# Attention, its fallback and the experts in one block instead of three, with the last tiles' work in another order

## The reference, cut to what matters

```python
def _attn_ref(q, k, v, f_logit):                 # (4, 8, 768, 48) each
    f = 1.0 / (1.0 + np.exp(-f_logit))
    for t in range(S):
        state = f[:, :, t, :, None] * state + np.einsum('bhd,bhe->bhde', k[:, :, t], v[:, :, t])
        y[:, :, t] = np.einsum('bhd,bhde->bhe', q[:, :, t], state)

def _moe_ref(x, modality_id, w_gate, modality_bias, w1, w2):   # x (3072, 384), 8 experts, F = 1024
    logits = x @ w_gate + modality_bias[modality_id]
    e_idx = np.argmax(logits, axis=1)
    ...
    for e in range(E):
        h = np.maximum(x[mask] @ w1[e], 0.0)
        out[mask] = gate_w[mask, None] * (h @ w2[e])

def _moe2_ref(x, w_gate, w_val, w_out, rms_g):   # d_ff = 1536
    xn = x / rms * rms_g
    g = xn @ w_gate
    silu = g * (1.0 / (1.0 + np.exp(-g)))
    return (silu * (xn @ w_val) @ w_out)
```

## Time and profile before

| | |
|---|---|
| median of three runs | 852.22 us |
| profiled execution, its own time | 848.39 us |
| its span (first to last instruction) | 846.6 us |
| PE busy | 815.0 us, 96% of the span |
| DVE, ACT, POOL busy | 452.4, 379.8, 138.3 us |
| mean granted TensorE clock | 0.988 of full speed |

### The profile page before, as it was taken

How to read it: one execution, slowest core, us unless ns; L and a number is a source line. 1 busy time by engine, 2 the same in 40 slices (tenths; PEclk the granted TensorE clock), 3 DMA queues, 4 the chain that set the end, 5 groups by cost and what they waited for, 6 DMA issues and landing times.

```text
span 846.6 us, 15716 instructions
## 1 busy us (share of the span) xinstructions
PE 815.0 (96%) x5624; PEld 740.5 (87%) x5624; DVE 452.4 (53%) x715; ACT 379.8 (45%) x742; POOL 138.3 (16%) x170
## 2 busy tenths in 40 slices
PE   6999987989999999989999999999999999999997
PEld 6888866989999999988889888888888888888887
DVE  7989894868776666644444343343333334333332
ACT  5999973746665555544223312232232233223222
POOL 4003042178660000010001100100020010001001
PEclk9999996999999999999999999999999999999999
DMA  9988874879878987622001000200100000000000
GB/s 184 201 161 210 178 232 145 289 272 353 290 226 254 317 297 245 217 58 94 0 1 57 19 2 1 74 0 0 37 37 0 0 37 0 0 0 37 0 0 37
DMA packets 44121, 96.59 MB, mean 114 GB/s; under 512 B 9200, under 2 KB 25072, under 8 KB 43952
## 3 DMA queue, kind: packets, MB, share of 16 engines
q1 hardware_dynamic: 39984, 85.81, 34.7%
q0 software_dynamic: 3840, 9.47, 3.1%
q10 hardware_dynamic: 256, 0.79, 0.4%
HBM read 76.75 MB, written 19.29 MB: 113 GB/s over the span
## 4 chain that ended last, share of the span: by engine, by line
PE 79%; issue 1%; DMA 1%; DVE 1%; POOL 0%; SPq 0%; ACT 0%; DVEq 0%; ACTq 0%
PE h_ps L1852 16%; PE h_ps L1853 16%; PE h_ps L1851 16%; PE ym_ps L1851 7%; PE ym_ps L1853 7%; PE ym_ps L1852 7%; PE xTm_ps L1851 3%; PE xTm_ps L1853 3%; PE xTm_ps L1852 3%; PE xT_ps L1868 1%; PE xTm_ps L1859 1%; DMA w_raw<-in_w 1%; POOL out L1533 0%; DMA x_regions<-zero_row 0%; DVE w_lo L1729 0%
## 5 line engine op out<-in xcount | busy, mean ns | idle before, releaser
L1826 DVE TENSOR_TENSOR gs<-h_ps,sig 128x512 f32<-128x512 f32 x72 | 49.8, 692 | 176.5 <-ACT sig L1640 176.5
L1640 ACT ACTIVATE sig<-h_ps 128x512 f32<-128x512 f32 x72 | 43.1, 598 | 159.7 <-PE h_ps L1853 159.7
L1651 ACT CAST h_hi<-hid 128x512 fp32r<-128x512 f32 x72 | 44.6, 620 | 150.2 <-DVE hid L1829 150.2
L1851 PE MATMUL h_ps<-x_hi,w_hi 128*128 128x256 f32 x312 | 89.7, 288 | 6.6 <-DVEq L1753 3.4
L1852 PE MATMUL h_ps<-x_hi,w_lo 128*128 128x256 f32 x312 | 89.3, 286 | 0.0
L1853 PE MATMUL h_ps<-x_lo,w_hi 128*128 128x256 f32 x312 | 89.3, 286 | 0.0
L1853 PE MATMUL h_ps<-w_lo,wg_hi 128*128 128x512 f32 x216 | 85.2, 394 | 0.0
L1852 PE MATMUL h_ps<-w_hi,wg_lo 128*128 128x512 f32 x216 | 85.0, 394 | 0.0
L1851 PE MATMUL h_ps<-w_hi,wg_hi 128*128 128x512 f32 x216 | 84.1, 389 | 0.0
L1853 PE MATMUL h_ps<-w_lo,wv_hi 128*128 128x512 f32 x216 | 84.1, 389 | 0.0
L1851 PE MATMUL h_ps<-w_hi,wv_hi 128*128 128x512 f32 x216 | 84.0, 389 | 0.0
(11 more groups left out here) (237 smaller groups left out, 1794.2 us busy)
## 6 DMA issues: line engine op xcount, KB each, us to landing
w_raw<-in_w SPq DMA_DIRECT2D x52, 384.0 KB, 5.1
w_in<-in_w SPq DMA_DIRECT2D x52, 384.0 KB, 5.4
qkf_in<-in_qkf SPq DMA_DIRECT2D x43, 288.0 KB, 5.0
y_sorted<-x_tiles SPq DMA_DIRECT2D x13, 384.0 KB, 3.3
v_in<-in_v SPq DMA_DIRECT2D x24, 192.0 KB, 5.3
x_regions<-zero_row SPq DMA_DIRECT2D x12, 384.0 KB, 3.1
x_tiles<-x_regions SPq DMA_DIRECT2D x12, 384.0 KB, 3.8
g_in<-in_wg SPq DMA_DIRECT2D x3, 768.0 KB, 7.2
```

Of the source, the lines that this page charges most:

```text
L1640: nc.scalar.activation(sig[:], g_ps, ACT.Sigmoid).then_inc(sig_done, 1)
L1651: nc.scalar.copy(h2_hi[:, fb % HELD], hid[:]).then_inc(h2_hi_done, 1)
L1826: nc.vector.tensor_tensor(gs[:], g_ps, sig[:], ALU.mult).then_inc(gs_done, 1)
L1851: nc.tensor.matmul(out, hi, rhs_hi, start=first, stop=False)
```

## The change

The three functions return their engine programs instead of opening a block each, and `build` opens one block in which every engine runs attention, the fallback and the experts one after another. A `Handover` object holds the semaphores that cross the borders. Where a barrier stood there are now waits: the engines wait for `own_steps` 4 before they load the flag; PE loads it ahead of its last x matmuls; SP waits in the experts for all logits (`x_kept` 24) and the scatters of tiles 16 to 19 (`ended`), DVE and POOL for `x_kept`, ACT for w2. In PSUM `h_ps` and `xT2_ps` change places. The other edits move work:

- the rows ahead are turned on PE behind the last y (`read` of tile 23) and the flag's matmul, and no longer in front of x of tile 21;
- SP asks for all four pieces of w2 behind the rows; before, two pieces were in front of them;
- `hi_w1` of piece 0 on ACT moves from step (5, 2) to (5, 3), and all later pieces behind the y copies; `lo_w1` and `lo_x` on DVE move behind the last `hold`;
- `KEPT_BY` lets tiles 10, 12, 14 and 15 be scattered one tile earlier, and tiles 18 and 19 without such a wait;
- at the start, `clamp` of tile 2 moves on DVE behind `kT` and `qT` of tile 1, `hold` of tile 0 goes ahead of `sums`, and on ACT the copy of the keys goes ahead of the logarithms;
- in the first expert tile `rows_of_tiles` and `gates_of_tokens` move on DVE from the end of the tile into its middle.

```diff
-        KEPT_BY = {2: 10, 3: 10, 4: 11, 5: 12, 6: 13, 7: 14, 8: 15, 9: 16, 10: 18, 11: 18, 12: 19, 13: 19, 14: 20, 15: 20, 18: 22, 19: 22}
+        KEPT_BY = {2: 10, 3: 10, 4: 11, 5: 12, 6: 13, 7: 14, 8: 15, 9: 16, 10: 17, 11: 18, 12: 18, 13: 19, 14: 19, 15: 19}
...
-            sp.wait_ge(y_done, NT - 3)
-            first.load_w2(sp, e, w2, ahead_sems, range(0, 2))
             for b in range(B):
                 sp.wait_ge(scattered[b], 16 * (LATE // B))
             sp.wait_ge(scattered_late, 16 * B)
             first.load_rows(sp, e, x_regions, ahead_sems)
-            first.load_w2(sp, e, w2, ahead_sems, range(2, GR))
+            first.load_w2(sp, e, w2, ahead_sems)
...
+    def flag_of(self, eng, flag):
+
+        eng.wait_ge(self.own_steps, self.FLAG_KNOWN)
+        return eng.value_load(flag[0:1, 0:1], min_val=0, max_val=1)
...
+            sp.wait_ge(shared.x_kept, NT)
+            sp.wait_ge(shared.ended, 16 * B)
...
                 if place == "first":
                     lo_w2(0, 3)
+                    rows_of_tiles()
                     next_w1(0)
...
                 lo_h(3)
                 if place == "first":
+                    gates_of_tokens()
                     next_w1(1)
                     next_w1(2)
...
-                if place == "first":
-                    rows_of_tiles()
-                    gates_of_tokens()
...
+        block = ctx.enter_context(nc.Block(no_gpsimd_drain=True))
+
+        @block.sync
+        def _(sp):
+            own.sync(sp)
+            general.sync(sp)
+            rest.sync(sp)
```

220 lines of the change are left out of this document (130 added, 90 removed).

## The result

The changed kernel takes **837.87 us** in the median of four runs (837.05 to 838.23), beside 852.17 us for the kernel before (850.54 to 854.04): 14.3 us less, a ratio of 0.983 (95% interval 0.9808 to 0.9852). In a second set, on another occasion, it took 840.8 us (six runs, 836.12 to 844.42) beside 851.88: 11.1 us less, ratio 0.987 (0.9832 to 0.9908). The two intervals overlap only at their ends: a median here tells no difference of 2 to 3 us from none. The forecast was 841.1 us, 11.1 us less.

A forecast was written before the change was run, and what follows sets the result against it. PE bounds the kernel, so time is won only where it waits or runs at a low clock. Terms 0.8 + 8.5 + 1.0 + 0.8 = 11.1 us gave a median of 841.1 us, range 836.5 to 846.5.

The forecast's parts named there:

- rival 1: Second and third tile: the collision stays away and the clock stays up, 14.8 us gained, 837.4 us; chance 0.15.
- the collision: Second and third tile: POOL's wg_lo runs over DVE's w_lo; a w_lo then took 3.96 us instead of 0.96.
- The start: First attention tiles on DVE: the first hold goes ahead of sums; 0.8 us gained, bounds 0 and 1.2.
- (a): End of attention: kT of tile 23 follows hold directly, as the late weight cast moves behind tile 23's factors; 1.1 us.
- (b): End of attention: PE no longer waits for the rows, runs 8.8 us at full clock, ends at 133.2 instead of 140.1.
- (c): Border from attention to routing on DVE: 1.2 us instead of 2.85; routing begins at 135.2, 8.5 us earlier.
- Rival 4: Border still costs 2.85 us instead of 1.2, because code behind the fallback must be fetched: 842.8 us; chance 0.06.
- (d): First expert tile: DVE's chain from routing to first h_lo stays 6.3 us; the second tile starts 8.5 us earlier.
- rival 2: First expert tile: the clock falls after PE's waits, 2.2 us less gain, 843.3 us; chance 0.12.
- The second and third tile: Ten small DVE steps leave the second tile's path, 1.0 us; the third tile's wait of 1.6 us moves, 0.8.
- rival 3: First expert tile: w2 asked for last lands late, ACT waits, h_lo ends 4.0 us later: 845.1 us; chance 0.06.

The follow-up runs named there:

- start_old: The changed kernel with the first tiles in the old order (sums ahead of the first hold, keys and clamp in their general places): 839.13 us.
- pad10: The changed kernel with 120 idle semaphore increments added to PE's queue, ten in each of 12 steps: 839.02 us.
- no_fallback: The changed kernel without the fallback's code and without the flag's load and test, on all engines: 839.32 us.
- pool_late: The changed kernel with GpSimd's wg_lo held until the second tile's first h_lo is done: 836.53 us.
- rows_old: The changed kernel with the rows of the tiles and the gates back at the end of the first tile's work on VectorE: 841.62 us.
- pool_no_fallback: The changed kernel with wg_lo held until the second tile's first h_lo and the fallback left out on every engine: 836.55 us.
- joined_pool: pool_late with two meeting points of all five engines, one behind the attention and one behind the fallback: 840.93 us.
- after_again: The changed kernel once more, with nothing changed, for a second set of runs and a second profile: 840.8 us.

## Why the prediction was right, and where it wasn't

The sum was 11.1 us; the profiled executions give 10.1 and the medians 14.3 and 11.1. Its terms were off in both directions and made up for each other: +0.9 at the start, -3.0 from there to the second tile's start, +2.1 in the second and third tile, -1.0 behind the sixth. That the sum came out is in good part luck. The first median is also beside it for another reason: the prediction took 3.8 us off both kernels for the way from the profiled execution to the median, and after had -0.4 in its first set (838.23 profiled, 837.87) and 2.5 in its second (838.28, 840.8). That 837.87 is near rival 1's 837.4 says nothing for rival 1: the collision came and the clock fell.

- **The start: 0.8 predicted, 1.7 measured** (a `hold` at 120.16 instead of 121.88), 1.9 by start_old, in executions without a loss elsewhere. The bound of 1.2 was wrong: it counted the first `hold` only. The clamps didn't wait for loads in after.
- **(a) and (b): right.** `kT` of tile 23 comes 2.9 us earlier, 1.72 of it from the start, 1.2 from the cast (1.1 predicted). From there to the last logits VectorE took 16.65 us before and 10.67 in after, 6.0 less; this is the largest single part, and it is read from the two profiles. PE runs from the scores to the last x without a wait at full clock, with one turn of the rows behind the last read, and ends at 131.15. 133.2 was predicted, less the start's 0.8: 132.4. In runs where w1 comes late the cast's new place gains more, which is part of why the medians moved by more than the profile.
- **(c): right on VectorE, missed on PE and on SyncE.** VectorE's border took 0.88 us idle (1.2 predicted, 2.85 before), and routing starts at 132.85 (134.4 predicted). PE's border of 4.46 us was not in the sum. Rival 4 named the cause, but put it on VectorE's path. The step that failed: "PE could begin 133.8"; with the start's 0.8 that is 133.0, and PE began at 135.61. A second step failed beside it: behind SP's wait for the scatters "only the first two loads of the dense weights are queued". The counts for which ScalarE's casts of w2 wait stand there too. In after this cost nothing (ScalarE then stood 3.47 us for PE), without the fallback 1.14 and 2.20 us on VectorE. The Trainium skill's page Runtime: NRT & Kernel Launch (Instruction fetch mechanics) says that a taken branch whose target is out of the loaded window stalls for a fetch. The runs agree in that the wait is there only with the code that is jumped over; they add that it can be absent with the branch in place (pad10). The DMA view of after, from 130 to 137 us, shows instructions being loaded; the columns are packets, MB and share:

```profile
q14 instruction: 3, 0.02, 1.0%
q8 instruction: 1, 0.02, 0.9%
```

  In no_fallback the first of the two rows is missing there. In pad10, where PE passes the branch at 134.3 us without a wait, both are there from 132 to 140 us, and neither from 133 to 135. That the wait is this fetch is likely, and not shown: no view ties a packet to the instruction that waits.
- **(d): the path was right, its length not.** The second tile's start was to come 9.3 us earlier with the start's part, and came 7.2 earlier (158.08 instead of 165.24). The step that failed is that the chain on DVE from the routing to the end of the first `h_lo` "will take the same", 6.3 us. It took 9.15 (132.85 to 142.00), because PE's late first block made its count late and VectorE stood 2.33 us for it. So of 10.85 us won at the routing 8.4 reached the first scatter, 7.8 the request for the second tile's rows, and 7.2 its start. The clock also fell: with PE idle from 131 to 135.6 the first 18 products ran at 0.21 us each instead of 0.12, 1.7 us together, which is rival 2 by another wait. Without the border's wait (no_fallback) the second tile comes only 1.2 us earlier, since VectorE then stands for w2's cast, the scatters take longer, and the clock falls for 15 products all the same. Behind the scatters come the rows' load and w1's third piece in SyncE's queue, with casts in that order on ScalarE.
- **The second and third tile: 1.8 predicted, 3.9 measured** (75.97 to 72.05 us for four tiles). The collision came where it was forecast, over the last `w_lo` of the second tile's weights: 5.84 us for four. It took 2.05 us (pool_late: 3.79), so 1.6 us in the tiles were lost to it. The Trainium skill's GPSIMD Engine Reference (Specifications) says that GpSimd shares its SBUF interfaces with VectorE, with contention where a VectorE instruction has two SBUF inputs; the trace agrees (`w_lo` has two and was held up, `h_lo` kept 0.68 us). The prediction's bound for the case that this contention decides, -0.9 for the second tile, was wrong: with the collision there the second tile still gained 2.35 and the third 1.50. It counted too little for the ten steps that went from the path. Back in their old place (rows_old) the tiles take 6.0 us more, of which 2.8 lie between the last `w_lo` and `h_lo`; I had priced the move at 2.0 to 3.9, from before's slack. The third tile's wait of 1.6 is gone, as forecast with half its size.
- **w2 last:** ScalarE waited 2.44 us at 134.11, put down to SyncE, whose count for w2 stands behind its wait for scatters. In after PE was later still, so rival 3 cost nothing. In pool_no_fallback ScalarE's wait was 4.28 us and put down to w2's load. This part was not undone by itself.
- **Not seen: 1.0 us behind the sixth tile** (607.5 before, 608.5 after). It is the clock in the last expert tile. It fell in nine of the twelve profiles of the changed order and its variants and in neither of the two of before; whether the change makes it likelier stays open.

Routing's 10.85 us add up as 1.7 from the start, 1.2 from the cast, 6.0 from the rest of the end of attention and 2.0 from VectorE's border. That one block in place of three is a small part of this is what joined_pool shows; that the new order at the end of attention is the large part is by subtraction.

## What to carry to other kernels

A stage that takes its steps at a fixed period (17.60 us here) is a ruler: read when it is entered and how long it takes to settle, and a change of 1 us can be placed that no median resolves. Read one event in two profiles of the same kernel first, as a measure of chance. Time won ahead of such a stage counts only as far as its first step's loads come earlier too; 4 us won on TensorE at the border were worth 1.2 at the next tile and nothing that can be seen at the end, since another wait, of work that stood ahead in VectorE's queue, came up behind it. And when small work is moved out of one engine's path, look where the work that it releases on a neighbour will run: holding GpSimd's six sets behind one more `h_lo` gave back what the move had cost.

## What the runs showed of the hardware

- A wait of 2.4 to 4.5 us on TensorE behind a jump over the fallback's code, in seven profiles with the same code of TensorE; none without that code and its flag (three profiles), and none with 120 fillers ahead of it (one). The same kernel had 4.46 and 2.87 us in two executions.
- VectorE with two SBUF inputs is held up by GpSimd with two: four `w_lo` of 128x768 took 3.79 us without `wg_lo` beside them and 5.84 beside three; a single one took 0.95 alone and 4.27. GpSimd's three `wg_lo` took 3.77 us where that single `w_lo` stood, and 5.79 beside the four. `h_lo`, which reads PSUM, kept 0.68 us.
- TensorE's clock was 1.00 until it stood without work for 4.46 us; the first 18 products behind that ran at half of full (1.2 GHz), and then it was 1.00 again. In no_fallback a wait of 1.36 us was followed by 15 such products, in pad10 one of 2.23 us by 27. In after_again the nine products right behind a wait of 2.87 us still ran at full, and the clock fell behind them.
- Behind a wait of 2.5 to 2.65 us ahead of the last expert tile the clock fell to half for 3 to 4 us in nine profiles and stayed full in five, and this is worth 0.7 to 1.0 us.
- Two executions of one program differed by 3.6 us at the end of attention and by nothing in the span.
